# Two orders of work changed in a fused attention and expert kernel: one VectorE step in every MLP block, and the sync queue's loads in the attention stage

## The reference, cut to what matters

```
q_p, k_p = phi(q), phi(k)                 # 4 batches, 8 heads, 576 tokens, head 64, 128 features each sign
den = einsum(q_p, sum(k_p)) + 1e-6
x   = einsum(q_p, k_p^T v) / den          # reshaped to 2304 tokens x 512
h   = x @ w_in                            # 512 -> 2048
y   = (h * clip(h + 3, 0, 6) / 6) @ w_out # 2048 -> 512
e   = argmax(y @ w_gate)                  # 8 experts, 1024 wide
out = gate * sigmoid(y @ w_output_gate)[e] * (relu(y @ w1[e]) @ w2[e])
```

## Time and profile before

| | |
|---|---|
| median of 3 runs | 822.21 us (821.75 to 822.86) |
| the profiled execution | 821.75 us, span 820.2 us |
| PE busy | 801.5 us (98%) |
| DVE busy | 557.4 us (68%) |
| ACT busy | 394.6 us (48%) |
| POOL busy | 182.3 us (22%) |
| mean granted TensorE clock | 0.996 of full speed |

### The profile page before, as it was taken

How to read it: one execution, slowest core, us unless ns; L and a number is a source line. 1 busy time by engine, 2 the same in 40 slices (tenths; PEclk the granted TensorE clock), 3 DMA queues, 4 the chain that set the end, 5 groups by cost and what they waited for, 6 DMA issues and landing times.

```text
span 820.2 us, 19359 instructions
## 1 busy us (share of the span) xinstructions
PE 801.5 (98%) x7080; PEld 497.8 (61%) x7081; DVE 557.4 (68%) x1144; ACT 394.6 (48%) x863; POOL 182.3 (22%) x210
## 2 busy tenths in 40 slices
PE   8999999999999999999999999999999999999995
PEld 6666666655555555555555555556767777777773
DVE  6788798878988988988898897845623453222221
ACT  6888899984655654754645645534101121010110
POOL 4456666660000011010010001010311232111000
PEclk9999999999999999999999999999999999999998
DMA  8567778746557657765765766383264826166600
GB/s 251 182 201 220 222 194 242 216 116 214 220 205 233 217 219 233 242 229 205 223 241 182 243 220 194 135 346 142 97 265 162 363 64 255 61 243 239 237 27 15
DMA packets 67454, 164.41 MB, mean 200 GB/s; under 512 B 28614, under 2 KB 32966, under 8 KB 60736
## 3 DMA queue, kind: packets, MB, share of 16 engines
q1 hardware_dynamic: 61472, 146.74, 52.8%
q0 software_dynamic: 5760, 16.80, 5.8%
q10 hardware_dynamic: 160, 0.07, 0.0%
HBM read 114.16 MB, written 47.55 MB: 197 GB/s over the span
## 4 chain that ended last, share of the span: by engine, by line
PE 63%; DVE 16%; issue 11%; POOL 5%; ACT 4%; DMA 1%; DVEq 0%; ACTq 0%; POOLq 0%
PE ps L939 13%; PE ps L928 12%; PE ps L1029 11%; PE ps L1041 11%; DVE u_mx L1608 4%; PE ps L750 3%; PE ps L782 3%; PE ps L815 3%; DVE arena L1633 3%; POOL arena L597 3%; DVE relu L1686 2%; PE ps L766 2%; DVE y_words L1600 2%; PE ps L824 1%; DVE stage L1691 1%
## 5 line engine op out<-in xcount | busy, mean ns | idle before, releaser
L928 PE MATMUL ps<-arena,w_in_sb 128*128 128x384 f16 x1152 | 200.9, 326 | 0.0
L939 PE MATMUL ps<-w_out_sb,arena 128*128 128x512 f16 x576 | 171.3, 379 | 1.9 <-DVE stage L1691 1.9
L928 PEld LDWEIGHTS ps<-arena,w_in_sb 128*128 128x128 f16 x1152 | 111.8, 98 | 81.1 <-issue 0.2
L1325 ACT ACTIVATE x_t<-ps 128x512 f16<-128x512 f32 x54 | 31.6, 596 | 199.3 <-PE ps L1029 174.0
L1029 PE MATMUL ps<-x_t,arena 128*128 128x128 f16 x2112 | 121.5, 219 | 1.7 <-issue 1.7
L1029 PEld LDWEIGHTS ps<-x_t,arena 128*128 128x128 f16 x2112 | 119.2, 98 | 5.5 <-issue 2.2
L1041 PE MATMUL ps<-arena,x_t 128*128 128x512 f16 x528 | 117.9, 379 | 0.0
L939 PE MATMUL ps<-w_out_sb,stage 128*128 128x512 f16 x288 | 109.1, 379 | 0.0
L1297 ACT ACTIVATE arena<-relu 128x384 f16<-128x384 f32 x96 | 50.0, 521 | 122.5 <-DVE relu L1686 122.3
L939 PEld LDWEIGHTS ps<-w_out_sb,arena 128*128 128x128 f16 x576 | 55.9, 98 | 61.9 <-issue 4.8
L1799 DVE SCALAR_TENSOR_TENSOR x_t<-ps,x_t 128x512 f16<-128x512 f32 x54 | 36.7, 689 | 78.2 <-ACT x_t L1325 75.9
(11 more groups left out here) (210 smaller groups left out, 906.1 us busy)
## 6 DMA issues: line engine op xcount, KB each, us to landing
arena<-split SPq DMA_DIRECT2D x36, 1024.0 KB
arena<-in_moe_w SPq DMA_DIRECT2D x16, 2048.0 KB, 12.9
split<-arena SPq DMA_DIRECT2D x16, 2048.0 KB, 7.5
arena<-in_qkt SPq DMA_DIRECT2D x15, 576.0 KB, 4.2
stage<-in_moe_w_in SPq DMA_DIRECT2D x16, 512.0 KB, 4.5
stage<-in_moe_w_out SPq DMA_DIRECT2D x16, 512.0 KB, 5.8
x_t<-rows POOLq DMA_DIRECT2D x27, 257.0 KB
y_words<-recs SPq DMA_DIRECT2D x32, 144.0 KB, 4.0
```

Of the source, the lines that this page charges most:

```text
L928: last = nc.tensor.matmul(ps[:, HB[f % GB], 0:BN], w_in_sb[:, lw, c, f * P:(f + 1) * P], xt[:, a, lx, c, :], start=c == 0 and lw + lx == 0 ...
L939: last = nc.tensor.matmul(ps[:, YB + r, :], g_sb[lg_][:, f % GB, r * P:(r + 1) * P], w_out_sb[:, lw, f, :], start=f == 0 and lg_ + lw == 0 ...
```

## The change

It has two parts that don't touch each other.

In the MLP blocks, chunk 3 is put into `SOON`. In all six blocks VectorE's order in chunk 3 is then `gate_chunk(3)`, `gate_lo(3)`, second `unit_search`; it was `gate_chunk(3)`, second `unit_search`, `gate_lo(3)`.

In SyncE's attention loop `next_v(u + 2)` goes ahead of the weight pieces, and the reading back of the reciprocals goes one round earlier and behind it: `rec_in(u - 3)` in the round that issued `rec_out(u - 3)`, where `rec_in(u - 4)` opened the round before. The `rec_in(12)` after the loop falls away, since round 15 does it.

```diff
-SOON = (0, 1, 2, FC - 1)
+SOON = (0, 1, 2, 3, FC - 1)
...
             for u in range(PAIRS):
-                if u > 3:
-                    rec_in(u - 4)
                 if u > 2:
                     rec_out(u - 3)
+                if u + 2 < PAIRS:
+                    next_v(u + 2)
+                if u > 2:
+                    rec_in(u - 3)
                 if 0 < u < PAIRS - 1:
                     next_pieces(u - 1)
-                if u + 2 < PAIRS:
-                    next_v(u + 2)
                 if u > 0:
                     den_over(u - 1)
...
-            rec_in(PAIRS - 4)
             sp.wait_ge(num_done, PAIRS)
```

## The result

The changed kernel takes **826.34 us** (median of 6 runs, 824.88 to 829.37) against 822.16 us of the kernel before (6 runs, 821.75 to 823.23). The ratio is 1.0059, 95% interval 1.0038 to 1.0080: 3.1 to 6.6 us slower. The forecast was 825.2 us, 3.0 us slower. The direction is right, and so is most of the size, but one of its two parts was put at nothing; alone it costs 1.0 us in the median, and over 3 us in some executions. The profiled execution is one of these: 828.33 us with a span of 826.7, 6.5 us longer than before.

The account below looks back on a forecast made before the run. VectorE's chain was taken to set the MLP blocks' pace, though TensorE looks full. Block 0's 0.53, 2.4 for blocks 1 to 4, block 5's 0.10 and 0 for the queue made 3.0 us: 822.2 to 825.2, range 823.3 to 826.5.

Parts of the forecast that it names:

- the waits of 1.9 us at output(3) go, and return larger at output(5): MLP block 3: TensorE's 0.62 us wait at output(3) comes back as 0.89 us at output(5).
- 0.67 us on VectorE's chain per block, 0.6 of it at TensorE: MLP blocks: 0.59 us idle plus 0.08 lost overlap lengthen VectorE's chain; blocks 1 to 4 lose 0.60 us each.
- rivals B: MLP block starts: VectorE has slack there, so only output(5) pays; about 1.8 us slower, 824.0 us; chance 0.10.
- E: MLP blocks: TensorE makes up the 0.6 us per block somewhere unseen; no change, 822.2 us; chance 0.07.
- rival C: VectorE's loop in the MLP: instruction fetch absorbs the short stalls; 2.3 us slower, 824.5 us; chance 0.10.
- rival A: MLP, output(3): TensorE's waits are simply removed; 1.9 us faster, 820.3 us; chance 0.07.
- I put this part at 0: SyncE's attention queue: earlier loads gain nothing and later ones still arrive in time; 0 us, or -0.3 to 2.
- landed 3.3 us later, about 77.4: no wait, the loads of v cover it: Attention round 6: store issued at 74.13 lands before rec_in(3) needs it; second piece lands 1.8 us ahead of need.
- next_v ahead of the pieces is hidden: SyncE's attention queue: no engine waits for these loads except at the start, so issuing next_v earlier gains nothing.
- Rival D: Attention, search at 88.35: pieces land about 2 us late; 5.0 us slower in all, 827.2 us; chance 0.06.
- The range, 823.3 to 826.5: Whole kernel time: the range of 8 in 10, with 0.6 us on either side for scatter.
- the forecast's own range: Whole kernel time around the forecast of 825.2 us: 824.6 to 825.9 us; chance 0.60.

Follow-up runs that it names:

- the split search: Against the kernel before, queue unchanged: in chunk 3 gate_lo(3) stands between the search's two reductions; 821.48 against 822.47 us, ratio 0.9993.

## Why the prediction was right and wrong, step by step

- **That the waits of 1.9 us at output(3) go, and return larger at output(5).** Right. In block 3, 1.05 us where 0.89 was forecast. In blocks 1 to 4 the waits are 0.58, 1.02, 1.05 and 0.85 where 0.8 to 1.1 was forecast, and all of TensorE's waits for `gate_lo` are 4.5 where it was about 5.
- **0.67 us on VectorE's chain per block, 0.6 of it at TensorE.** Right, and a little small: 0.71 in block 3, and the MLP is 3.3 us longer, in the whole change and alone, where the sum gave 3.0. Block 0 is 0.54 (forecast 0.53), block 5 0.11 (0.10), and blocks 1 to 4 are 2.69 together (2.4). With that rivals B, 1.2 us for the four blocks, and E are out. The stall at the start of block 3, 0.36 before, is 0.55 in the trace after (VectorE's row maximum at 376.56) and 0.69 in that of VectorE's part alone. That is 0.2 to 0.3 us more, the size of the difference, but kernels with the old order of chunk 3 also differ in their MLP by up to 0.7 us (373.5 to 374.2), so it isn't shown that this is the cause. The row before names TensorE as what ended the 0.36; but its last matmul ended at 370.89, before VectorE was free at 370.94, and what the stall is stays open.
- **That the instruction stalls might take it up (rival C).** Wrong. The 0.35 within `unit_scale` of block 2 is there in the trace after with 0.35 as well. The rule of the Trainium skill (Runtime: NRT & Kernel Launch, Instruction fetch mechanics) that instructions are fetched ahead would have allowed for it. The 0.35 did not shrink behind the longer idle time.
- **That TensorE's waits are what can be won (rival A).** Wrong, shown by the split search, which removes the five waits and is not measurably faster. The Trainium skill (Perfetto Trace Analysis, Identifying the Most-Contended Engine) goes by the highest occupancy, which is TensorE's 98%. But it adds what the prediction left out, that for TensorE the room left is to be judged by other measures, among them the busy share of its weight loads, which is 61% here. In this stage it is the chain of VectorE, 68% busy, that sets the blocks' length.
- **"I put this part at 0."** This is the step that failed, and in it the landing of the store, "landed 3.3 us later, about 77.4: no wait, the loads of v cover it". In round 6 itself the read-back goes out 6.6 us behind the store, 0.7 us after the last load of v was issued, and the search of the round's piece waits:

```profile
74.26 0.33 SPq L418 DMA_DIRECT2D recs<-rec  x1
...
80.89 1.10 SPq L434 DMA_DIRECT2D y_words<-recs  x2
```

```profile
88.77 1.22 DVE L1411 TENSOR_REDUCE w_mx<-stage 128x1 f32<-128x1024 f32 x1 [0.21 <-DMA stage<-in_moe_w_out]
```

From 92 us on the store lands after 7.3 us in the median. The 3.3 came from a queue in which the last big loads stood further ahead: in round 6 the last piece was issued 8.6 us and the load of q and k 2.7 us ahead of the store, and they are 3.1 and 1.9 us ahead of it in the trace after, and 1.0 us for q and k in round 13. The change removes that distance, and I kept the old duration. In round 13 SyncE stands 4.4 us; in round 14, 6.7. A store's issue, 7 us of landing and 3.8 us of issues behind the read-back's start make a round of 11.5 us, longer than a pair, and the lag adds up over the last rounds. I had looked at the tightest piece of one round (1.8 us of margin, all of it gone) and not at what the round's length does to the next.
- **That next_v ahead of the pieces is hidden.** Right, by itself: no difference.
- **Rival D**, pieces late by 2 us, had the reader right in the trace after: VectorE waits 0.8 and 1.9 us for them. It had the place wrong: it put them at the search of round 6, and they stand at 159 and 172 us. It had 0.06, and deserved more.
- **The range, 823.3 to 826.5.** That 826.34 lies inside it is luck. Its upper end is that of the forecast's own range with 0.6 us for scatter, and nothing for the queue; what fills it is the queue part, and three of the six runs lie above it.

## What to carry to other kernels

When a full engine waits in short regular pieces for another, look at whether the other one has any slack from one block to the next; if it has none, its chain is the bound, and an order that takes away the waits but adds idle time to that chain loses. Put work between a step and the answer that it waits for, rather than the wait itself. And a small transfer's landing time can hang on what was issued ahead of it: when an issue is moved, the landing is to be read again with its new neighbours, and a queue's round is to be summed and held against the stage's pace.

## What the runs showed of the hardware

With chunks 3 and 4 both early, TensorE waits 3.12 us in front of output(5) of block 2, and then runs at half its clock for a few microseconds. In this stretch of its timeline a matmul group at 340.23 takes 1.06 us, and the same form at 344.96, below, 0.59:

```profile
339.39 0.62 PE L939 MATMUL ps<-w_out_sb,arena 128*128 128x512 f16 x2 [3.12 <-DVE stage L1691]
...
340.23 1.06 PE L939 MATMUL ps<-w_out_sb,arena 128*128 128x512 f16 x2
...
344.96 0.59 PE L939 MATMUL ps<-w_out_sb,arena 128*128 128x512 f16 x2
```

From the start of output(5) to that of output(6) it is 344.96 - 339.39 = 5.6 us, where it is 3.9 in the kernel before. The granted clock from 339 to 349 us is 0.83 in the view by stretches, which is part of the stretch at 1.2 GHz and the rest at 2.4:

```profile
339.00:349.00 10.00, 9.61 (x43) 4.70 (x44) 9.85 (x14) 4.58 (x7) 0.00 (x0) 0.83 0.61 221
```

The same happens in block 4 behind a shorter wait, again with 5.6 us to the next output (471.93 to 477.50) and a granted clock of 0.83 from 472 to 482:

```profile
471.93 0.59 PE L939 MATMUL ps<-w_out_sb,arena 128*128 128x512 f16 x2 [2.05 <-DVE stage L1691]
```

After the waits of 1.71 us (block 1) and 2.30 us (block 3) of the same kernel the clock stays at 1.00. So the length of the wait alone does not decide it: 2.05 us was followed by the lower clock and 2.30 us was not. None of the waits that the change itself adds is over 1.7 us, and its granted clock is 1.00 from 20 to 560 us. It means that a wait can cost more than its length, here about 1.7 us more each for those of 3.12 and 2.05 (0.17 of 10 us).
